# Who copies and loads the first batch's value sums in an attention and feed-forward kernel

## The reference, cut to what matters

```python
k_sum = k.reshape(B, H, nb, block, D).max(axis=3)        # block 32, nb 24
v_sum = v.reshape(B, H, nb, block, D).mean(axis=3)
scores_l = scale * q @ k.T        where |i - j| < 16, else -1e9
scores_s = scale * q @ k_sum.T + log(block)
a = softmax(concatenate([scores_l, scores_s]))
x = a @ concatenate([v, v_sum])                          # 1536 tokens x 512
x = (silu(x @ w_gate) * (x @ w_val)) @ w_out             # inner width 1536
h = x @ w_in                                             # inner width 2048
out = where(h >= 1, h, where(h <= -1, 0, (h + 1)**2 / 4)) @ w_out2
```

## Time and profile before

| what | value |
|---|---|
| median of 3 runs | 614.23 us (613.68 to 614.72) |
| the profiled execution | 614.17 us |
| its span | 612.4 us |
| PE busy | 588.3 us, 96% |
| DVE busy | 469.8 us, 77% |
| ACT busy | 365.1 us, 60% |
| POOL busy | 87.2 us, 14% |
| DMA | 59.77 MB, mean 98 GB/s |

### The profile page before, as it was taken

The page is one execution under the profiler, slowest core; times in us unless marked ns, Lnnn a source line. Parts: engine busy times, 40 slices in busy tenths (PEclk is TensorE's granted clock), DMA queues, the critical chain, the costliest instruction groups (busy, mean ns, idle before and its releaser), DMA issues.

```text
span 612.4 us, 10207 instructions
## 1 busy us (share of the span) xinstructions
PE 588.3 (96%) x3720; PEld 539.3 (88%) x3720; DVE 469.8 (77%) x914; ACT 365.1 (60%) x735; POOL 87.2 (14%) x78
## 2 busy tenths in 40 slices
PE   2889999999999999999999999999999999999997
PEld 2466789999899999999999999998878899998886
DVE  6578698888866757888766757997998479979843
ACT  4883888988755445556645445665565356665522
POOL 4452134333310002222210000000000000000000
PEclk9989999999999999999999999999999999999999
DMA  9998235334112202223212202321211323011212
GB/s 330 290 284 265 84 109 146 106 113 147 36 52 69 70 1 71 81 88 123 86 36 70 70 1 68 130 87 59 69 52 52 138 70 118 4 36 69 70 52 103
DMA packets 32961, 59.77 MB, mean 98 GB/s; under 512 B 3280, under 2 KB 7376, under 8 KB 32912
## 3 DMA queue, kind: packets, MB, share of 16 engines
q1 hardware_dynamic: 32384, 58.21, 29.9%
q10 hardware_dynamic: 528, 0.92, 0.6%
HBM read 54.53 MB, written 3.15 MB: 94 GB/s over the span
## 4 chain that ended last, share of the span: by engine, by line
PE 80%; DVE 9%; SPq 3%; DMA 3%; issue 2%; ACT 2%; POOL 0%; ACTq 0%; POOLq 0%; DVEq 0%
PE ps L526 45%; PE ps L663 17%; PE ps L635 15%; DMA k_raw_b<-k_t_dram 3%; DVE hid_lo L1165 1%; SPq L380 1%; PE ps L516 1%; PE ps L487 1%; DVE rel L1171 1%; DVE x_lo L1097 1%; DVE h L1174 1%; SPq L359 1%; PE ps L494 1%; DVE t_first L1089 1%; DVE t_late L1089 1%
## 5 line engine op out<-in xcount | busy, mean ns | idle before, releaser
L526 PE MATMUL ps<-x_hi,w_hi 128*128 128x384 f32 x560 | 191.2, 341 | 2.6 <-ACT part L862 1.4
L526 PE MATMUL ps<-x_lo,w_hi 128*128 128x384 f32 x560 | 187.4, 335 | 0.0
L526 PE MATMUL ps<-x_hi,w_lo 128*128 128x384 f32 x560 | 187.3, 334 | 0.0
L526 PEld LDWEIGHTS ps<-x_hi,w_hi 128*128 128x128 f32 x560 | 105.1, 188 | 6.8 <-issue 5.0
L526 PEld LDWEIGHTS ps<-x_hi,w_lo 128*128 128x128 f32 x560 | 105.2, 188 | 0.4 <-issue 0.2
L526 PEld LDWEIGHTS ps<-x_lo,w_hi 128*128 128x128 f32 x560 | 105.1, 188 | 0.0
L896 ACT ACTIVATE wout_hi<-wout_raw 128x512 fp32r<-128x512 f32 x56 | 35.3, 631 | 95.1 <-PE ps L663 52.0
L663 PE MATMUL ps<-wout_hi,hid_hi 128*128 128x512 f32 x192 | 74.8, 390 | 0.8 <-DVE wout_lo L1159 0.8
L663 PE MATMUL ps<-wout_hi,hid_lo 128*128 128x512 f32 x192 | 75.2, 392 | 0.1
L663 PE MATMUL ps<-wout_lo,hid_hi 128*128 128x512 f32 x192 | 74.8, 390 | 0.0
L1159 DVE TENSOR_TENSOR wout_lo<-wout_raw,wout_hi 128x512 fp32r<-128x512 f32 x56 | 39.4, 704 | 40.1 <-ACT wout_hi L896 39.6
(11 more groups left out here) (105 smaller groups left out, 917.6 us busy)
## 6 DMA issues: line engine op xcount, KB each, us to landing
w_raw<-w_dram SPq DMA_DIRECT2D x80, 256.0 KB, 2.9
wout_raw<-w_dram SPq DMA_DIRECT2D x56, 256.0 KB, 2.6
out_dram<-y_out SPq DMA_DIRECT2D x12, 256.0 KB, 2.1
k_a<-k_t_dram SPq DMA_DIRECT2D x6, 384.0 KB, 7.0
v_s<-v_rows_dram SPq DMA_DIRECT2D x6, 384.0 KB, 15.0
v_a<-v_rows_dram SPq DMA_DIRECT2D x6, 384.0 KB, 4.5
k_raw<-k_t_dram SPq DMA_DIRECT2D x3, 512.0 KB, 4.6
q_a<-q_t_dram SPq DMA_DIRECT2D x6, 256.0 KB, 6.8
```

The costliest lines, as they stand in the source:

```text
L526: last = nc.tensor.matmul(dst, lhs, rhs, start=start and kk == 0 and i == 0, stop=kk == 1 and i == 2, skip_group_check=not start)
```

## The change

It takes the two copies from the bank of value sums and the three loads out of ACT's program. The copies go to DVE, which does them after the inverses of tile 5 (in iteration 6 of its loop). The loads go to SP, which issues them after value pair 5 and ahead of the second batch's three key loads; before the first, SP waits for the first copy.

```diff
@@ SP
+            def place_first_sums(j):
+                if j == 0:
+                    sp.wait_ge(v_sum_ready, 1)
+                c0, c1 = SUMS_AT[j]
+                sp.dma_start(v_s[WIN:, c0:c1], v_sum[WIN:, 0].unsqueeze(1).to_broadcast([P - WIN, c1 - c0, DM])
+                             ).then_inc(v_first_sums[j], 16)
+
@@
             load_v(4)
             load_v(5)
+            for j in range(len(SUMS_AT)):
+                place_first_sums(j)
             for c in range(3):
                 load_k_raw(1, c)
@@ ACT
-            def place_first_sums():
-                nc.scalar.activation(v_s[WIN:, 0:2], v_sum_ps[0][WIN:, :].unsqueeze(1).to_broadcast([P - WIN, 2, DM]),
-                                     ACT.Copy).then_inc(v_pair_sums, 1)
-                act.wait_ge(v_sum_ready, 1)
-                for j, (c0, c1) in enumerate(SUMS_AT):
-                    act.dma_start(v_s[WIN:, c0:c1], v_sum[WIN:, 0].unsqueeze(1).to_broadcast([P - WIN, c1 - c0, DM])
-                                  ).then_inc(v_first_sums[j], 16)
-
@@
                 if s == 3:
                     w_hi_s(0)
-                elif s == 5:
-                    copy_v_sum(0)
-                    place_first_sums()
@@ DVE
+            def place_v_sum():
+                dve.wait_ge(v_sum_done, 1)
+                nc.vector.tensor_copy(v_sum[WIN:, 0], v_sum_ps[0][WIN:, :]).then_inc(v_sum_ready, 1)
+                nc.vector.tensor_copy(v_s[WIN:, 0:2], v_sum_ps[0][WIN:, :].unsqueeze(1).to_broadcast([P - WIN, 2, DM])
+                                      ).then_inc(v_pair_sums, 1)
+
@@
                 elif s == 4:
                     w_lo_s(0)
+                elif s == 6:
+                    place_v_sum()
```

## The result

| | before | with the change |
|---|---|---|
| median of 6 runs | 614.16 us (613.68 to 615.51) | 619.93 us (617.92 to 620.6) |
| profiled execution, its span | 614.17 us, 612.4 us | 620.07 us, 618.4 us |
| mean granted clock over the span | 0.994 | 0.992 |

The ratio is 1.0093 with a 95% interval of 1.0082 to 1.0104: slower by 0.93%; the medians are 5.8 us apart. The forecast was 618.6 us, with 615.4 to 621.2 as its range.

The account below looks back on a forecast made before the run. PE, busy 96% of the span, was taken as the bound, with first-stage delays passing to the end. Sums late behind SP's line plus a halved clock shift the maxima 4.35 us: 614.17 + 4.4 = 618.6 us, range 615.4 to 621.2.

Parts of the forecast that it names:

- The line on SP: SP's queue, backed up some 18 us: loads land in issue order, so sums land behind the last value pair.
- Step 1: PE at values 2: stands from 31.6 until the first sums land at 37.8, starts at 38.0, +2.7 us.
- Step 2: PE after that idle: clock halved some 6.2 us; six groups from values 2 end at 44.3.
- its case with the clock kept: Clock does not fall: tiles 2 and 3 at ACT's pace, maxima at 42.75, shift 1.65 us, 615.8 us.
- Step 3: Values 4 from 44.3, copied by DVE; second batch's key maxima start at 45.45, not 41.10: +4.35 us.
- Step 4: After the maxima: same DVE work, PE and ACT about as late, so +4.4 us reaches the end: 618.6 us.
- DVE's copies: Ahead of tile 7's mask: 0.6 and 1.15 us on DVE, absorbed by its idle and the loads' wait.
- The keys: `k_raw_b` loads on SP: issued 6.3 us later, yet still landing at 41.1 to about 43.6.
- The clock stays: Rival at PE's wait: sums land late but the clock is kept; slower, 615.8 us, chance 0.13.
- The queue doesn't matter: Rival: sums land 8 to 10 us after issue on SP too; no change, 614.2 us, chance 0.09.
- the line is emptied while SP waits: Rival: DMA engines run out between 22.4 and 28.7, keys land late; 618.6 to 621.5 us, chance 0.08.
- ACT's freed time wins: Rival at values 2: early sums and keys move the maxima by up to 3.7 us; 610.5 us, chance 0.04.

Follow-up runs that it names:

- experiment 2: Changed kernel with the three loads of sums back on ACT's queue, after tile 6's exponentials, copies still on DVE: 616.0 us, ratio 1.003.
- experiment 3: Changed kernel with SP's three key loads ahead of the three loads of sums: 624.12 us, ratio 1.0167.
- experiment 6: Changed kernel with SP's three loads of sums ahead of value pairs 4 and 5: 616.21 us, ratio 1.0024.
- experiment 9: The changed kernel itself, measured again on another chip: 619.51 us, ratio 1.0082.
- filled profiles: Changed kernel with unused matmuls on PE ahead of values 2: 14 of them 622.26 us; 7 of them 618.76 us, repeated 617.16 us.
- experiment 1: Changed kernel with both copies back on ACT, the three loads still on SP's queue: 618.66 us, ratio 1.0079.
- experiment 8: Kernel before, with POOL issuing the sums' loads, DVE copying for tiles 0 and 1, keys ahead of value pairs 4 and 5: 613.01 us, ratio 0.9972.
- experiment 12: The version of experiment 8 (POOL loads, keys first) again, beside experiment 11: 613.48 us, ratio 0.9987.
- experiment 10: Changed kernel with 7 filling matmuls on PE ahead of values 2, repeated beside experiment 9: 617.16 us, ratio 1.0052.
- experiment 5: Changed kernel with 7 filling matmuls on PE ahead of values 2, first run: 618.76 us, ratio 1.0074.
- experiment 11: As experiment 8, but with SP's order of the kernel before (value pairs 4 and 5, then keys): 615.12 us, ratio 1.0016.

## Why the prediction was right, and where its size was off

- **The line on SP.** Right: the sums landed in issue order, behind value pair 5 and ahead of the keys. Experiments 2, 3 and 6 move the landing by moving either the queue or what stands ahead, at the same time of issue.
- **Step 1, the mis-sized term.** It had the first load land at 37.8 and PE wait 6.3 us; it landed at 39.3, and PE waited 7.34. The step that failed is "40.0 - 2.7 = 37.3" for value pair 5: this landed at 38.6, only 1.4 earlier. That ACT's loads were ahead of the pair was right, since all three had landed by 37.5. Wrong was to give back their 2.7 us of transfer in full: without them the 16 DMA engines were as busy (1.07 for 1.06) but moved less in each us, 254 GB/s up to the pair's landing for 270 before. Why is not shown. The first load of sums then took 0.7 us behind it, not 0.5. Values 2 started at 39.56 for 38.0: 1.56 us, more than the 1.3 us by which the median missed the forecast. The stretch up to the pair's landing, in the kernel before and in the changed one (columns as in the earlier trace rows):

```profile
22.42:40.00 17.58, 14.81 (x206) 10.34 (x204) 9.13 (x72) 14.49 (x58) 6.24 (x6) 0.81 1.06 270
22.42:38.60 16.18, 8.38 (x120) 5.40 (x119) 8.47 (x54) 10.42 (x45) 5.51 (x6) 0.90 1.07 254
```

- **Step 2, the clock.** Right in the profile of the changed kernel: 6.22 us from values 2 to values 4 for a predicted 6.3, at half the clock. That the 6.2 us of the dip before came again is in part luck: in experiment 9, the same kernel, the clock was back 3.8 us after work resumed. The clock's worth is shown by the 5.0 us of the filled profiles against 6.55 to 7.42: 1.5 to 2.4 us, where the prediction had 2.7 (45.45 less the 42.75 of its case with the clock kept), since it had 4.75 us for what takes 5.0 at full clock, and 7.45 for what took 7.29.
- **Step 3.** Values 4 to maxima: 1.07 us for a predicted 1.15. The start of the maxima is 46.85 for 45.45, which is the 1.56 of step 1 less some tenths.
- **Step 4.** The delay goes to the end: predicted 4.35 and 4.4, measured 5.75 and 6.0.
- **DVE's copies.** 0.70 and 1.22 us (0.62 from start to start for the first); predicted 0.6 and 1.15. They do hold PE up, by 1.34 us ahead of values 0, and the mask of tile 7, which follows them at 28.42; `v_pair_sums` came at 28.39 for a predicted 27.9. All of this is over before PE stands at values 2 for 7.34 us, so it doesn't reach the time: experiment 1 without them is within 1.3 us of the changed kernel on another chip, and by the table the difference is in the maxima's start, 0.9 us, of which 0.3 are the earlier start of values 2 and 0.6 come behind it, where the clock rose earlier.
- **The keys.** Predicted at 41.1 as before; they landed at 42.8, in a window in which the engines moved less (263 GB/s between 22.42 and 41.07 against 278 in the earlier trace rows, at the same share of 1.06). That cost nothing, since DVE came to them at 46.85.
- **The rivals.** "The clock stays" would have needed PE's wait to leave it at 1.00; it fell. "The queue doesn't matter" fell in experiment 2; "the line is emptied while SP waits" did not happen: the share of the DMA engines was 1.06 up to 41.07. "ACT's freed time wins" needs both early sums and early keys, and experiments 8 and 12 have that: it is worth 0.1% to 0.3%, not the 3.7 us of its bound.

## What to carry to other kernels

In all these profiles the landing of a small load (128 KB) was set by what stood ahead of it in its queue: with the same time of issue it took 8.3, 12.0 or 16.9 us by its place on SP's queue. So read the time from issue to landing of its neighbours before moving a load to another queue. A small, urgent load that is issued late belongs on a queue other than the one with the bulk, or ahead of the bulk whose turn comes later. When PE has to stand, add to the wait what the halved clock may cost afterwards (here 1.5 to 2.4 us). Work that fills the wait, even useless work, can win that back, but only if it ends by the time the load lands: 7 matmuls did so in experiment 10 and overran it by 1.5 us in 5, and 14 made the changed kernel slower still. And what leaves a queue need not give back its transfer time in full.

## What was not expected of the hardware

The clock's return was not tied to a fixed time of work: in the same kernel, after waits of 7.34 and 6.91 us, it took 6.0 us in one profile and 3.8 in the other. Nor did the length of PE's wait decide alone whether the clock fell: 2.36 us cost it in the kernel before, 2.49 us in experiment 11 did not, and in experiment 12, after 2.89 us, it fell 1.6 us after the work had resumed (PE and the windows around the resumption, experiment 11 and then 12).

```profile
34.95 0.69 PE L516 MATMUL ps<-prob_ts,v_s 128*64 128x64 f32 x16 [2.49 <-DMA v_s<-v_sum]
36.50:37.00 0.50, 0.50 (x11) 0.33 (x11) 0.50 (x7) 0.14 (x1) 0.00 (x0) 1.00 1.05 246
```
```profile
34.96 0.69 PE L516 MATMUL ps<-prob_ts,v_s 128*64 128x64 f32 x16 [2.89 <-DMA v_s<-v_sum]
36.50:37.00 0.50, 0.50 (x5) 0.18 (x5) 0.50 (x7) 0.00 (x0) 0.00 (x0) 0.54 1.00 254
```

A DMA issued by POOL in a full line overtook SP's queue as ACT's did (7.4 to 8.2 us to the first landing, against 12.0), and its three issues took 1.9 us. DMA engines at a share of 1.06 moved between 223 and 278 GB/s, so a share row alone doesn't give the time that a load needs; the term of step 1 was worked out from such a row.
